# Attention scores from each head's 64 array rows, in 128-query tiles, ahead of a woven MLP

## The reference

```
scores = where(causal, -1e9, q @ k.T / 8);  a = exp(scores - max);  a /= a.sum + 1e-9
mem    = (phi(q) @ M_prev) / (phi(q) @ z_prev + 1e-6)      # phi(x) = relu(x) + exp(min(x, 0))
attn   = g * mem + (1 - g) * (a @ v),  g = sigmoid(beta[head])
h = x @ w_in [512, 2048];  x = (h * sigmoid(h)) @ w_out
h = x @ w2_in [512, 1024]; s = h * softmax(h); ln = layernorm(s) * g_ln; out = ln @ w2_out
```

## Time and profile before

| | us |
|---|---|
| runs: median (lowest to highest), 3 runs | 905.37 (904.7 to 907.11) |
| the profiled execution, its own time | 907.41 |
| its span in the profile | 905.6 |
| attention alone: first matmul to first MLP matmul | 10.4 to 113.4 |
| attention and MLP woven | 113.4 to about 543.6 |
| last 768 tokens, second MLP | 543.6 to 905.6 |
| TensorE (PE) busy | 858.3 |
| VectorE (DVE), ScalarE (ACT), GpSimd (POOL) busy | 548.7, 422.5, 356.8 |

### The profile page before, as it was taken

How to read it: one execution, slowest core, us unless ns; L and a number is a source line. 1 busy time by engine, 2 the same in 40 slices (tenths; PEclk the granted TensorE clock), 3 DMA queues, 4 the chain that set the end, 5 groups by cost and what they waited for, 6 DMA issues and landing times.

```text
span 905.6 us, 13741 instructions
## 1 busy us (share of the span) xinstructions
PE 858.3 (95%) x4736; PEld 749.9 (83%) x4736; DVE 548.7 (61%) x1216; ACT 422.5 (47%) x928; POOL 356.8 (39%) x367
## 2 busy tenths in 40 slices
PE   4788799999999999999999999999998999999996
PEld 3777688888888888888888879999997888888885
DVE  6888775887775566575565533144425666666663
ACT  4777657766655645556655434334111222222221
POOL 5777657767645446455555224133110000000000
PEclk9888889999999999999999999999998999999999
DMA  5222245666655444544444337434300000000000
GB/s 167 76 66 72 85 145 200 212 207 234 230 182 170 164 140 145 175 141 147 146 150 147 109 130 304 137 117 139 118 0 1 24 23 23 23 23 23 23 24 23
DMA packets 48042, 105.64 MB, mean 117 GB/s; under 512 B 7536, under 2 KB 18800, under 8 KB 47728
## 3 DMA queue, kind: packets, MB, share of 16 engines
q1 hardware_dynamic: 47984, 104.89, 34.6%
HBM read 83.37 MB, written 21.50 MB: 116 GB/s over the span
## 4 chain that ended last, share of the span: by engine, by line
PE 64%; issue 25%; DVE 5%; ACT 2%; POOL 1%; DMA 1%; SPq 1%; POOLq 0%; ACTq 0%
PE banks L1245 23%; PE banks L1257 20%; PE banks L1213 9%; PE banks L1165 7%; PE banks L1193 5%; DVE pt_lo L914 1%; DVE phi L881 1%; PE banks L1371 1%; DVE neg_max L901 1%; POOL st L645 1%; DVE xc_lo L932 1%; PE banks L1168 1%; DMA z_row<-in_z_prev 1%; ACT pt_hi L667 0%; DVE k_lo L876 0%
## 5 line engine op out<-in xcount | busy, mean ns | idle before, releaser
L1257 PE MATMUL banks<-g_hi,wr 128*128 128x512 f32 (+1 forms) x640 | 196.7, 375 | 1.1 <-POOL g_lo L546 0.8
L1245 PE MATMUL banks<-xc_hi,wr 128*128 128x512 f32 x384 | 133.7, 409 | 4.1 <-DVE xc_lo L932 4.1
L1257 PEld LDWEIGHTS banks<-g_hi,wr 128*128 128x128 f32 x640 | 118.6, 188 | 15.7 <-issue 1.6
L524 POOL TENSOR_SCALAR prob<-prob,inv_sum,gate_all 128x576 f32<-128x576 f32 (+2 forms) x144 | 97.8, 681 | 70.5 <-DVE inv_sum L908 68.1
L667 ACT ACTIVATE pt_hi<-banks 128x512 fp32r<-128x512 f32 (+2 forms) x160 | 77.7, 490 | 94.2 <-PE banks L1193 93.0
L1257 PE MATMUL banks<-g_lo,wr 128*128 128x512 f32 (+1 forms) x320 | 117.8, 368 | 0.0
L901 DVE TENSOR_REDUCE neg_max<-banks 128x1 f32<-128x576 f32 (+2 forms) x144 | 69.7, 484 | 66.7 <-PE banks L1168 66.0
L542 POOL TENSOR_TENSOR g_lo<-gu,g_hi 128x512 fp32r<-128x512 f32 x48 | 62.0, 1291 | 111.6 <-ACT g_hi L711 111.5
L914 DVE TENSOR_TENSOR pt_lo<-banks,pt_hi 128x512 fp32r<-128x512 f32 (+2 forms) x160 | 86.9, 547 | 17.0 <-ACT pt_hi L667 16.3
L645 POOL TENSOR_TENSOR st<-st 128x1 f32<-128x1 f32 x18 | 9.9, 549 | 218.5 <-DVE st L1096 218.5
L1213 PE MATMUL banks<-pt_hi,vm 128*128 128x320 f32 (+4 forms) x352 | 92.0, 292 | 2.0 <-issue 1.2
(11 more groups left out here) (110 smaller groups left out, 1910.9 us busy)
## 6 DMA issues: line engine op xcount, KB each, us to landing
wr<-split_w SPq DMA_DIRECT2D x96, 512.0 KB, 3.3
split_w<-wr SPq DMA_DIRECT2D x32, 512.0 KB, 4.4
q_raw<-in_q_t SPq DMA_DIRECT2D x16, 288.0 KB, 2.8
k_raw<-in_k_t SPq DMA_DIRECT2D x16, 288.0 KB, 3.2
qn_raw<-in_q_n SPq DMA_DIRECT2D x16, 288.0 KB, 3.5
out<-o SPq DMA_DIRECT2D x18, 256.0 KB, 2.0
vm_raw<-in_v_main SPq DMA_DIRECT2D x16, 256.0 KB, 2.6
wr_raw<-in_w_in SPq DMA_DIRECT2D x16, 256.0 KB, 4.3
```

The source lines that it names most:

```text
L524: pool.tensor_scalar(pr, pr, inv_sum[p % 2][:, t:t + 1], gate_all[:, source(p), 1:2], ALU.mult, ALU.mult)\
L1245: mm = pe.matmul(out_bank, w[:, a, k], x[:, k], start=(i == 0), stop=(i == 3 * KC - 1))
L1257: mm = pe.matmul(out_bank, w[:, a, k], g, start=(i == 0), stop=(i == 11))
```

## The change

Nine score tiles of 64 queries of both heads become five: the tail tile t = 4 (`TAIL`) holds the last 64 queries of both heads block-diagonally, as before, and tiles t = 3 to 0 hold 128 queries of each head. For these, a head's scores are a matmul over its own 64 partitions only (`q[r, ...]`, `k[r, ...]`), each head into a PSUM bank of its own, and the heads take turns, matmul by matmul. q needs no block-diagonal copy but for the tail: `q_raw` is 640 columns wide, with the tail block zeroed and loaded in two further DMAs. There are five row maxima (over two banks) for nine, still nine exps and nine scalings, five pairs of 1/sum operations for eight, nine transpose units for ten (with as many transposes), one split of q on ScalarE and one on GpSimd for two each. The key range of a tile is now a multiple of 128.

Score tiles fall on steps 0, 1, 3, 5 and 7 of a pair, in banks 0-1 and 5-6 by turns while attention is alone, and in banks 0-1 only when woven. The tables for exps, sums, turns and units are new. At the beginning, VectorE zeroes the tail block, `phi`'s last block and `vm_raw` instead of GpSimd and of the `qd` buffers, the first `q_lo` is made by VectorE, beta is loaded from ScalarE's queue in four DMAs behind which stands a small copy, its first activation. `first_pass` takes the first four weight units in the last 16 steps before 44, not 8. The chunk's four blocks of `x_t` are split as their pairs end: `X_BEFORE` puts them 4, 3, 1 and 1 steps ahead of the chunk, and each waits for its own pair only.

```diff
+SCORES = {0: 4, 1: 3, 3: 2, 5: 1, 7: 0}
+TILES = [4, 3, 2, 1, 0]
+EXPS = [(4, 0), (3, 0), (3, 1), (2, 0), (2, 1), (1, 0), (1, 1), (0, 0), (0, 1)]
+EXP_ALONE = [2, 3, 3, 5, 5, 7, 7, 9, 9]
+EXP_WOVEN = [1, 2, 2, 4, 4, 6, 7, 8, 8]
+SUM_ALONE = [3, 4, 6, 9, 11]
+SUM_WOVEN = [3, 4, 6, 8, 10]
-UNITS = ["8a", "8b", "7", "6", "5", "phi", "4", "3", "2", "10"]
+UNITS = ["8a", "8b", "30", "31", "20", "21", "phi", "1", "0"]
-TURN = [[], [-4], [-3, -2], [], [-1], [0], [1], [2, 3], [4, 5]]
+TURN = [[], [-3], [], [-2], [-1], [0], [1], [2, 3], [4, 5]]
-SCORES_ALONE = ({8: 0, 7: 5, 6: 6, 5: 0, 4: 1, 3: 5, 2: 6, 1: 0, 0: 1}, {8: 5, 7: 0, 6: 1, 5: 5, 4: 6, 3: 0, 2: 1, 1: 5, 0: 6})
-SCORES_WOVEN = {8: 0, 7: 0, 6: 1, 5: 0, 4: 1, 3: 0, 2: 1, 1: 0, 0: 1}
+SCORES_ALONE = (0, 5)
+SCORES_WOVEN = 0
+X_BEFORE = [4, 3, 1, 1]
...
             def scores(p, t):
...
-                for b, lo, hi in spans:
-                    for n, (q, k) in enumerate(((qd_hi, k_hi), (qd_lo, k_hi), (qd_hi, k_lo))):
-                        mm = pe.matmul(b[:, 0:hi - lo], q[i][:, t], k[i][:, lo:hi], start=(n == 0),
-                                       stop=(n == 2 and hi < w), skip_group_check=True)
-                    if hi == w:
-                        mm = pe.matmul(b[:, hi - lo - D:hi - lo], ident_b[:], mask_b[:], start=False, stop=True,
+                products = ((q_hi[i], k_hi[i]), (q_lo[i], k_hi[i]), (q_hi[i], k_lo[i]))
+                if t < TAIL:
+                    w = P * (t + 1)
+                    for n, (q, k) in enumerate(products):
+                        for h in range(2):
+                            r = slice(h * D, (h + 1) * D)
+                            pe.matmul(bank[b + h][:, 0:w], q[r, P * t:P * (t + 1)], k[r, 0:w], start=(n == 0), stop=False,
+                                      skip_group_check=True)
+                    for h in range(2):
+                        mm = pe.matmul(bank[b + h][:, P * t:w], ident_b[:], mask_b[:, D:D + P], start=False, stop=True,
...
+                else:
+                    for half in range(2):
+                        for n, (q, k) in enumerate(products):
+                            pe.matmul(bank[b + half][:, 0:HALF], q[:, TQ:TQ + P], k[:, half * HALF:(half + 1) * HALF],
...
             def row_max(p, t):
...
+                if t < TAIL:
+                    dve.tensor_reduce(neg_max[p % 2][:, 2 * t:2 * t + 2], banks[:, b:b + 2, 0:P * (t + 1)], AX.X, ALU.max,
+                                      negate=True).then_inc(max_done, 1)
...
             def load_qk(p):
...
-                sp.dma_start(q_raw[:], q_t[i]).then_inc(qk_in, 16)
-                sp.dma_start(k_raw[:], k_t[i]).then_inc(qk_in, 16)
+                sp.dma_start(q_raw[:, 0:TQ], q_t[i, :, 0:TQ]).then_inc(q_in, 16)
+                sp.dma_start(k_raw[:], k_t[i]).then_inc(k_in, 16)
+                if not p:
+                    sp.wait_ge(q_zeroed, 1)
+                for h in range(2):
+                    sp.dma_start(q_raw[h * D:(h + 1) * D, TQ + h * D:TQ + (h + 1) * D], q_t[i, h * D:(h + 1) * D, TQ:S])\
+                        .then_inc(q_in, 16)
...
             def q_high(p):
...
-                for h in range(2):
-                    r = slice(h * D, (h + 1) * D)
-                    act.activation(qd_hi[sel(p)][r, :, h * D:(h + 1) * D], q_raw[r].rearrange("p (t c) -> p t c", t=NT),
-                                   ACT.Copy).then_inc(q_hi_done, 1)
+                act.activation(q_hi[sel(p)][:], q_raw[:], ACT.Copy).then_inc(q_hi_done, 1)
...
             def xc_high(c, k):
-                act.wait_ge(x_done, 4 * ALONE * (c + 1))
+                act.wait_ge(x_done, 4 * (ALONE * c + k + 1))
...
-            act.wait_ge(zeros_done, 2)
+            for h in range(2):
+                act.dma_start(beta_row[h * D:(h + 1) * D, 0], beta[h:h + 1, :].broadcast_to([D, NP])).then_inc(beta_in, 16)
+                act.dma_start(beta_row[:, 1 + h], beta[h:h + 1, :].broadcast_to([P, NP])).then_inc(beta_in, 16)
+            act.wait_ge(zeros_done, 1)
+            act.activation(phi[1][:, NT:NT + 1], phi[0][:, NT:NT + 1], ACT.Copy).then_inc(zeros_done, 1)
             q_high(0)
...
             k_high(0)
             k_low(0)
...
+            dve.wait_ge(q_hi_done, 1)
+            dve.tensor_tensor(q_lo[0][:], q_raw[:], q_hi[0][:].bitcast(F32), ALU.subtract).then_inc(q_split, 1)
+            phi_one(0)
```

More of the change, by code:

```diff
@@ L128, in scores_free, with columns, p_at @@
-    return 0
+    for n in range(tile_count(p, t) - 2, -1, -1):
+        q, u = n // len(TILES), TILES[n % len(TILES)]
+        if score_bank(q, u) == score_bank(p, t):
+            return NE * q + EXPS_AFTER[u]
+    return 0
+def columns(t, h):
+    return slice(8, 9) if t == TAIL else slice(2 * t + h, 2 * t + h + 1)
 def nblocks(t):
-    return t // 2 + 1
-def p_at(t):
-    return sum(nblocks(x) for x in range(t))
+    return t + 1
+def p_at(t, h):
+    return t * (t + 1) + h * (t + 1)
 def unit_place(pt, unit):
+    both = pt[:].rearrange("p h n c -> p n h c")
@@ L170, in units_of, with low_units_of @@
     return [(q, u) for q, u in both if 0 <= q < NP]
+def low_units_of(s):
+    return [pu for x in range(max(s - 3, 0), s + 1) for pu in units_of(x)
+            if (x + 0 if x + 0 < FIRST else max(FIRST, x + 0)) == s]
 def values_of(s):
@@ L616, in _ @@
-                if pair_at(s, -1):
-                    phi_times_z(pair_at(s, -1))
-                if pair_at(s, 2) is not None:
-                    phi_last(pair_at(s, 2))
-                    n_phi = pair_at(s, 2) + 1
-                for part, k in enumerate((8, 9)):
+                if pair_at(s, 4, 1):
+                    q_low(pair_at(s, 4, 1))
+                if pair_at(s, -2):
+                    phi_times_z(pair_at(s, -2))
+                if pair_at(s, 3) is not None:
+                    phi_last(pair_at(s, 3))
@@ new lines, in _ @@
+            for s in range(FIRST, LASTSTEP):
+                w = woven(s - 1)
+                for q, t in sums_of(s):
+                    for h in range(1 if t == TAIL else 2):
+                        normalise(q, t, h)
+                if w and MLP[w[1]][0] == "H":
+                    g_low(h_index(w[0], MLP[w[1]][1]))
+                if pair_at(s, -2):
+                    phi_times_z(pair_at(s, -2))
+                if pair_at(s, 3) is not None:
+                    phi_last(pair_at(s, 3))
+                for part, k in enumerate((7, 9)):
+                    if pair_at(s, k) is not None:
+                        v_low(pair_at(s, k), part)
+                if first_pass(s) is not None and MLP[first_pass(s)][0] == "H":
+                    w_low(first_pass(s))
+                if pair_at(s, 4, 1):
+                    q_low(pair_at(s, 4, 1))
@@ L1329, in _ @@
                     values(*values_of(s))
+                for q, u in turns[1:]:
+                    turn(q, u)
             for s in range(FIRST, LASTSTEP):
@@ L1334, in _ @@
                     turn(*turns[0])
-                if turns[1:]:
-                    turn(*turns[1])
+                for q, u in turns[1:]:
+                    turn(q, u)
                 if woven(s):
```

443 lines of the change are left out of this document (193 added, 250 removed).

## The result

| | before | after |
|---|---|---|
| median of the runs, us | 906.24 (4 runs) | 893.04 (890.32 to 897.84, 4 runs) |
| ratio to before, 95% interval | | 0.9858, [0.9827, 0.9889] |
| the profiled execution, own time; span | 907.4; 905.6 | 890.3; 888.5 |
| first matmul starts at | 10.4 | 8.3 |
| first MLP matmul starts at | 113.4 | 107.9 |

The change brings 13.2 us by the medians (10.1 to 15.7 by the interval), of 15.4 forecast. The profiled execution of the changed kernel is the fastest of its four, so the spans differ by more, 17.1: 5.5 before the first MLP matmul, 11.2 in the woven stage and 0.4 behind it. That is not how I had shared it out.

A forecast was written before the change was run, and what follows sets the result against it. TensorE's summed work bounds the woven stage; with attention alone, a ring of waits with VectorE longest. -3 - 6 - 2.5 - 4 = -15.5 from 907.4 gives 891.9, median 890; range 873 to 905.

The forecast's parts named there:

- Woven scores: TensorE's score matmuls in the woven stage, eleven pairs: -3 us, with ends -21 and +24.
- shares that differ: Woven score costs beyond the equal 5.4 us sums: overlap of two heads' streams, overlap of loads, and array changes.
- streams overlapped and loads queued: Woven scores: two heads' matmuls stream together but weight loads queue, 2.72 in place of 3.82 us, a gain of 1.1.
- bound 0 to 0.27 for a change: Woven tiles: each full-to-half array change costs between nothing and 0.27 us; 0.1 taken, 8 changes a pair.
- first rival: Everything overlaps and array changes cost 0.05 us: woven stage -17, the rest -12.5, giving 876; chance 0.2.
- Chunk heads: First MLP matmuls of a chunk no longer wait for x's split: -2 first, -1 each other, -4 us in all.
- The beginning: Kernel start: first matmul 3.2 us earlier, near 7.1, then z's second load in the way; -2.5 us counted.
- Attention alone: Stage before the MLP, VectorE the longest in the ring of waits: -5 us, and -1 from spread weight splits.
- Count 1.2 of the 1.45 as gained: With attention alone, VectorE saves 1.45 us a pair, 1.2 of it gained; four pairs' worth give -5.
- 1 for the weights: First weight splits, spread over 16 steps before the MLP, cost less of a jam: -1 us.
- 3 us either way: With attention alone, a less dense TensorE may see the half clock more: 3 us kept as uncertainty.

The follow-up runs named there:

- the part alone in the kernel before: Kernel before with only the chunk's four blocks of x split 4, 3, 1 and 1 steps ahead, each after its own pair: ratio 0.9937.
- fill: Changed kernel plus four bf16 matmuls of zeros per 128-query tile, pairs 0 to 4: 889.4 us, ratio 0.9805; two per tile in kernel before: 0.9977.
- with about 4: Changed kernel with beta's loads in SyncE's queue and eight bf16 matmuls of zeros a tile while attention is alone: 898.2 us, ratio 0.9912.
- full-array run: Changed kernel with score matmuls of tiles 3 to 0 on all 128 rows, not a head's 64 (scores summed over both heads): 893.9 us, ratio 0.9846.

## Why the prediction was right, point by point

**Woven scores: right in direction, too small.** The account of the work holds: full-array, the new tiles cost what the old ones did (5.4 and 5.4 in the sum, 35.8 and 35.8 in the traces). Of the shares that differ I took "streams overlapped and loads queued" and 0.1 us a change. The loads overlap as well, a gain of 1.9 and not 1.1, and a change costs 0.14: 1.9 - 8 x 0.14 = 0.8, against 0.7 measured for a pair, some 7 to 8 us in all and not 3. The step that failed is the mis-sized term for the loads, a gain of 1.1 where the loads' overlap makes it 1.9; of the bound 0 to 0.27 for a change, the value lay in the middle. This is the first rival's overlap at nearly three times its price for a change. The Trainium skill's TensorEngine Tiling (Array Packing), section Key Properties, had both halves: that tiles load and multiply in parallel, and that a change of mode drains. The trace agrees with both, 0.12 us for a couple of 256 columns and 0.28 us a tile.

**Chunk heads: right in size, in part by another way.** -4 forecast, 3.3 to 8.2 measured by the part alone in the kernel before. The waits of 4.1 us went, but the 2 us of the first head did not bring the first MLP matmul forward; in the profile a full clock in the first unit stood in for them.

**The beginning: -2.5 forecast; about -3.6 in the profile**, where the third pair's k split stands at 32.8 for 36.4. The first matmul came at 8.3 and not 7.1, since beta's loads beside q's were not in my sum.

**Attention alone: wrong.** "Count 1.2 of the 1.45 as gained", and 1 for the weights: -6. In the profile the three pairs from there on gained 0.2, 0.7 and 1.2 us, 2 in all, and the last stretch lost 0.2. Even these 2 us are mostly the clock's, since at the full clock both kernels take some 18.4 us a pair. The step that failed is taking VectorE, the longest in the round, for what sets its pace; the run without the eps additions shows that it isn't. The saving was too large as well: 1.45 in the sum, 0.5 to 0.7 in the windows. Part of that is the eps addition, priced at 0.15, which takes 0.42 on the mean in the changed kernel's pairs; why, no run shows. No effect of the weights' spread was seen. What the round waits for instead is not settled: with about 2 us of fill (and beta's loads moved; TensorE busy 16.4 for 14.3) the pairs stay at 18.4 and 18.6, with about 4 (18.0) they take 19.3, so TensorE's work is on it beyond some 3 us of slack; and no single wait in the lists is long.

**The clock: "3 us either way".** It is where the medians went. By the profiled execution the change is worth 17.1, by the medians 13.2. The full-array run shows it most: 7 us worse when woven, equal in the median, its executions' granted clock 0.981 to 0.990 for 0.962 to 0.981. A reason that fits is that scores from half the array leave TensorE with less to do while attention is alone: in a pair at the full clock it is busy 14.3 us, 15.1 with the full array and 16.4 with the fill. But the kernel before, busy 15.9 at a clock of 0.91, had 0.970 to 0.983 in its executions, so the busy time alone does not put the clocks in order. That the clock costs time is shown as far as the fill goes (3 us between medians of one set, with higher clocks in the executions, and 2 us in the kernel before); how much of the full-array run's return it explains was not separated.

So the sum came out near by luck: the woven term was 4 to 5 us too small, and the term for attention alone at least 4 too large.

## What to carry to other kernels

Two heads of 64 rows each can share the array at almost no cost in ordering, but each way between half and full array costs some 0.14 us here: put as many short matmuls as possible between two changes. Before counting an engine's saved work as time, take some away and look; being the longest in a ring of waits, 16.6 us of 19.3 here, does not make it the bound. Compare stretches at the same granted clock before calling a difference a gain. And where TensorE waits for others, a little work that changes nothing may pay by its clock, as two of these runs show; too much of it costs.

## What the runs showed of the hardware that I had not expected

- Matmuls of the two row halves overlap out of the order in which they are issued: three of head 0 and then three of head 1 were recorded as three couples, the middle one 0.17 us to the next for 384 columns, and a woven pair of heads took 35.1 us either way (one execution).
- The weight loads of two row halves overlap: a couple of 128x256 matmuls 0.12 us, where two loads in a row take 0.22.
- Going from the full to the half array and back costs 0.28 us a tile of 256 keys: 0.09 ahead of the first couple, 0.10 in it and 0.09 behind the last. With the full array throughout, none of the three is there.
- Matmuls of zeros added while attention is alone went with a higher granted clock: 0.981 to 0.988 over six whole executions, where sixteen without them had 0.962 to 0.985; in the kernel before 0.981 to 0.987 over twelve, 0.970 to 0.983 without.
- A pair alone at the full clock took 18.3 to 18.7 us in five kernels whose TensorE was busy from 14.3 to 16.8 us in it.
